# Attention and mixers in one block: the first mixer's matrix multiplies started in the last attention tiles, a second plain pair, spread seam transposes

## What is computed

```python
q_assign = argmax(einsum('bhsd,hcd->bhsc', q_n, c_n)); k_assign = argmax(... k_n ...)
scores = where(q_assign == k_assign, scale * q @ k.T, -1e9)       # B=2, H=8, S=768, D=64, 16 clusters
x = softmax(scores) @ v                                            # then [B, S, 512]
# first mixer (rank 32, hidden 2048)
u = x + (xT @ U @ V).T ;  x = u + relu(u @ w_ch1) @ w_ch2
# second mixer (token width 256, hidden 1536)
u = x + (relu(xT @ w_tok1) @ w_tok2).T ;  out = u + relu(u @ w_ch1) @ w_ch2
```

## Time and profile before

| | |
|---|---|
| median of 3 runs | 805.26 us (804.04 to 806.67) |
| profiled execution | 807.81 us, span 806.0 us |
| PE busy | 760.1 us (94%) |
| DVE, ACT, POOL busy | 555.3, 383.0, 229.7 us |
| mean granted PE clock | 0.989 of full |

### The profile page before, as it was taken

How to read it: one execution, slowest core, us unless ns; L and a number is a source line. 1 busy time by engine, 2 the same in 40 slices (tenths; PEclk the granted TensorE clock), 3 DMA queues, 4 the chain that set the end, 5 groups by cost and what they waited for, 6 DMA issues and landing times.

```text
span 806.0 us, 12514 instructions
## 1 busy us (share of the span) xinstructions
PE 760.1 (94%) x4189; PEld 680.9 (84%) x4189; DVE 555.3 (69%) x876; ACT 383.0 (48%) x709; POOL 229.7 (29%) x258
## 2 busy tenths in 40 slices
PE   6889999999999769999989999999899999889998
PEld 6778999999999659888978788988688888678987
...
DMA packets 64043, 66.65 MB, mean 83 GB/s; under 512 B 6400, under 2 KB 53824, under 8 KB 64000
## 3 DMA queue, kind: packets, MB, share of 16 engines
...
## 4 chain that ended last, share of the span: by engine, by line
PE 58%; DVE 4%; ACT 3%; issue 1%; ACTq 0%
PE bank L1193 27%; PE bank L1176 21%; PE bank L1157 3%; PE bank L1124 2%; PE bank L1109 2%; PE bank L1140 1%; ACT uT L1259 1%; DVE a_lo L1372 1%; ACT bc_hi L1252 1%; DVE x L1385 1%; DVE bc_lo L1395 0%; DVE w_lo L1424 0%; ACT a_hi L1245 0%; PE bank L1096 0%; DVE kT_hi L1429 0%
## 5 line engine op out<-in xcount | busy, mean ns | idle before, releaser
L1292 ACT ACTIVATE qT_hi<-h 128x768 fp32r<-128x768 f32 x48 | 40.6, 847 | 281.6 <-DVE h L1439 223.4
L1193 PE MATMUL bank<-w_hi,qT_hi 128*128 128x512 f32 x336 | 132.4, 394 | 1.8 <-DVE x L1380 1.7
L1193 PE MATMUL bank<-w_hi,kT_hi 128*128 128x512 f32 x336 | 133.4, 397 | 0.0
L1193 PE MATMUL bank<-w_lo,qT_hi 128*128 128x512 f32 x336 | 132.7, 395 | 0.0
L1176 PE MATMUL bank<-bc_hi,a_hi 128*128 128x384 f32 x336 | 112.4, 335 | 3.0 <-DVE kT_hi L1411 1.7
L1176 PE MATMUL bank<-bc_lo,a_hi 128*128 128x384 f32 x336 | 113.1, 337 | 0.0
L1176 PE MATMUL bank<-bc_hi,a_lo 128*128 128x384 f32 x336 | 112.3, 334 | 0.0
L629 DVE TENSOR_TENSOR pT_lo<-back,pT_hi 128x384 fp32r<-128x384 f32 x192 | 98.0, 552 | 6.7 <-ACT pT_hi L530 3.5
L530 ACT ACTIVATE pT_hi<-back 128x384 fp32r<-128x384 f32 x192 | 84.3, 497 | 35.6 <-PE back L774 33.6
L1031 POOL TENSOR_TENSOR a_raw<-a_raw 128x256 f32<-128x256 f32 x24 | 20.5, 856 | 282.5 <-DMA a_raw<-in_moe_w_ch_dram 281.3
L1439 DVE TENSOR_TENSOR h<-bank,h 128x384 f32<-128x384 f32 x120 | 64.4, 553 | 51.1 <-PE bank L1176 50.9
...
## 6 DMA issues: line engine op xcount, KB each, us to landing
...
```

Of the source, the lines that this page charges most:

```text
L1193: last = nc.tensor.matmul(acc[k][:, :], y[:, e, k * P:(k + 1) * P], w[n % 2][:, e, :], start=(start and i == 0), stop=(stop and i == 2))
L1292: nc.scalar.activation(hs_hi[:, e, :], h[:, e, :], ACT.Relu).then_inc(hs_hi_made, 1)
```

## The change

All of it in one block: `attention` and `mixers` now return one function for each engine, which `program` calls one behind the other, so that nothing joins the engines between them. Semaphores live as long as the block. `U_st` (the split U) has a place of its own. The mixers' parts for ACT, DVE and PE are cut into `head`, `middle`, `tail` and `rest`; the first ones are called inside the attention's last tiles (`mix`). The diff, cut to its core:

```diff
+        if last and t == TPP - 2:
+            steps.append(("MIX", 0, 0))
     if last:
-        steps += [("F", GPP - 2, 0)] + [("AV", GPP - 1, part) for part in range(AV_PARTS)] + [("F", GPP - 1, 0)]
+        steps += [("F", GPP - 2, 0), ("MIX", 1, 0)] + [("AV", GPP - 1, part) for part in range(AV_PARTS)]
+        steps += [("MIX", 2, 0), ("F", GPP - 1, 0)]
...
-                                pool.wait_ge(head_in[j], PAIRS * HEAD_LOADS)
-                        if G > 0:
+                                pool.wait_ge(head_in[j], (PAIRS if g is NPAIR - 3 else NPAIR - 2) * HEAD_LOADS)
+                            if g is NPAIR - 2:
+                                pool.wait_ge(uv_in, 5 * 16)
+                                split_V()
+                        else:
                             split_x(0, (g - NPAIR + 3) * GT + G - 1)
                     if last_pair:
                         if G == 0:
                             for j in range(2):
                                 pool.wait_ge(head_in[j], NPAIR * HEAD_LOADS)
-                            pool.wait_ge(uv_in, 5 * 16)
                             split_U()
-                        elif G == 1:
-                            split_V()
                         else:
-                            if G == 2:
+                            if G == 1:
                                 pool.wait_ge(x_done, (NPAIR - 1) * GPP)
-                            for i in range(GT * (G - 2), GT * (G - 1)):
+                            for i in range(2 * G - 2, 2 * G):
                                 split_x(1, i)
...
+                    if last_pair and t == TPP - 2:
+                        mix[0]()
                 if last_pair:
                     fin(GPP - 2)
+                    mix[1]()
...
+                    if last_pair and t == TPP - 1:
+                        mix[0]()
                     low(t, 0)
                     low(t, 1)
                     if first_pair and t == 0:
                         first_link(LAST)
                 if last_pair:
+                    mix[1]()
                     group(GPP - 1)
...
+    PLAIN = (2, 1, 1, 1)
...
-            return acc[t - 2] if cc == 0 and t >= 2 else ring_bank(cc, t)
+            return acc[t] if cc == 0 else ring_bank(cc, t)
...
-                if n == 1:
+                if n == 2:
...
-            pair_sums(1)
+            pool.wait_ge(tok_mm, B)
...
+                    pe.wait_ge(uT_made, t + 1)
+                elif t == 2:
+                    pe.wait_ge(exp_done, NPAIR * TPP)
+                elif t == 4:
+                    pe.wait_ge(p_lo, NPAIR * TPP * 2)
...
+                if p > 0 or g >= 2:
+                    pe.wait_ge(group_made, plain_at(n) + g - 1)
+                elif cc > 0:
+                    pe.wait_ge(uT_made, cc * NT + NT - 1 + g)
+                elif g == 0:
+                    pe.wait_ge(p_lo, NPAIR * TPP * 2)
                 else:
-                    pe.wait_ge(group_made, 4 * cc + g - 1)
+                    pe.wait_ge(fin_copied, NPAIR * GPP)
...
-                if start and k == 0:
-                    wait(pe, y_made, cc * NT)
-                    pe.wait_ge(u_made, min(cc + 2, NCH) * NT)
+                if start:
+                    wait(pe, y_made, (cc - 1) * NT + k + 1)
+                    pe.wait_ge(u_made, NT + k + 1 if cc == 0 else min(cc + 2, NCH) * NT)
...
+            def head():
+                token_first_low(0)
+
+            def middle():
+                for t in range(GT):
+                    token_second_low(0, t)
+
+            def tail():
+                for t in range(GT):
+                    transpose_u(0, t)
+                for t in range(GT, NT):
+                    token_second_low(0, t)
+
+            def rest():
+                group(0, 0, 0)
+                for t in range(GT, NT):
+                    transpose_u(0, t)
+                group(0, 0, 1)
+                token_first_low(1)
+                group(0, 0, 2)
+                for t in range(GT):
+                    token_second_low(1, t)
+                group(0, 0, 3)
+                for t in range(GT, NT):
+                    token_second_low(1, t)
+                for cc in range(NCH):
+                    if cc > 0:
+                        for g in range(len(GROUPS)):
+                            group(cc, 0, g)
+                            if cc in MIXED:
+                                for t in ((), (0,), (1, 2), (3, 4, 5))[g]:
+                                    token_first(cc, t)
+                    for p in range(1, PLAIN[cc]):
+                        for g in range(len(GROUPS)):
+                            group(cc, p, g)
+                            for unit in range(3 * g, 3 * g + 3):
+                                down(cc, p - 1, unit)
+                    for p in range(PLAIN[cc], npair[cc]):
+                        mixing = cc in MIXED and p == PLAIN[cc]
+                        units = iter(range(len(UNITS)))
+                        for q in range(BLOCKS):
+                            product(cc, p, q)
+                            if mixing and q == 1:
+                                for t in range(NT):
+                                    token_second(cc, t)
+                            if q > int(mixing):
+                                for unit in [next(units) for _ in range(4 if mixing and q == BLOCKS - 1 else 2)]:
+                                    down(cc, p - 1, unit)
+                    for unit in range(len(UNITS)):
+                        if cc + 1 < NCH:
+                            for t in {0: (0, 1), 2: (2,), 4: (3,), 6: (4,), 8: (5,)}.get(unit, ()):
+                                transpose_u(cc + 1, t)
+                        down(cc, npair[cc] - 1, unit)
+
+            return head, middle, tail, rest
...
+            def head():
+                a_high(0)
+                t1_high(0)
+
+            def tail():
+                for t in range(GT):
+                    block_high(0, t)
+
+            def rest():
+                for t in range(GT):
+                    uT_copy(0, t)
+                late = slice(DM - 2 * D, DM)
+                act.wait_ge(x_done, NPAIR * GPP)
+                nc.scalar.activation(x_hi[:, NT:2 * NT, late], x[:, :, DM + late.start:DM + late.stop],
+                                     ACT.Copy).then_inc(x_hi_made, 1)
+                group_high(0, 0)
+                for t in range(GT, NT):
+                    block_high(0, t)
+                group_high(0, 1)
+                a_high(1)
+                t1_high(1)
+                for t in range(GT, NT):
+                    uT_copy(0, t)
+                group_high(0, 2)
+                group_high(0, 3)
+                for e in range(2):
+                    w2_high(0, e)
+                group_high(0, 0, 1)
+                t_high(0, 0)
+                group_high(0, 1, 1)
+                t_high(0, 1)
+                for e in range(2):
+                    w2_high(1, e)
+                group_high(0, 2, 1)
+                t_high(0, 2)
+                a_high(2)
+                group_high(0, 3, 1)
+                t_high(0, 3)
+                for cc in range(NCH):
...
-                    t_high(cc, 0)
-                    t_high(cc, 1)
-                    group_high(cc, 0)
-                    a_high(n + 1)
-                    t_high(cc, 2)
-                    group_high(cc, 1)
                     for e in range(2):
                         w2_high(n, e)
+                    a_high(n + 1)
+                    group_high(cc, 0)
+                    t_high(cc, 0)
+                    group_high(cc, 1)
+                    t_high(cc, 1)
                     group_high(cc, 2)
+                    t_high(cc, 2)
                     group_high(cc, 3)
                     t_high(cc, 3)
...
+            def head():
+                a_low(0, 0)
+                t1_low(0)
+
+            def tail():
+                for t in range(GT):
+                    add_mix(0, t)
+
+            def rest():
+                for t in range(GT):
+                    block_low(0, t)
+                for t in range(GT, NT):
+                    add_mix(0, t)
+                late = slice(DM - 2 * D, DM)
+                dve.wait_ge(x_hi_made, 1)
+                nc.vector.tensor_tensor(x_lo[:, NT:2 * NT, late], x[:, :, DM + late.start:DM + late.stop],
+                                        x_hi[:, NT:2 * NT, late].bitcast(F32), ALU.subtract).then_inc(x_made, 1)
+                group_low(0, 0)
+                for t in range(GT, NT):
+                    block_low(0, t)
+                group_low(0, 1)
+                a_low(1, 0)
+                t1_low(1)
+                group_low(0, 2)
+                for t in range(GT):
+                    add_mix(1, t)
+                group_low(0, 3)
+                for t in range(GT, NT):
+                    add_mix(1, t)
+                w2_low(0)
+                group_low(0, 0, 1)
```

(25 more changed lines are left out.)

426 lines of the change are left out of this document (193 added, 233 removed).

## The result

The changed kernel takes 796.92 us in the median of four runs (795.7 to 797.63), the kernel before 805.24 beside it: ratio 0.9894, 95% interval 0.9872 to 0.9916. The change saves 8 to 10 us. The forecast was 788.8, with 784 to 796 as its range: the sign was right, the size was twice what came.

What follows compares the result with a forecast made beforehand. PE was taken to be bound by waits between attention and first woven pair, and at the seams. Savings of 12.6 + 1.8 + 0.4 + 1.7 = 16.5 us from 807.81, less 2.55 for the median, gave 788.8; range 784 to 796.

Steps and rivals of the forecast that it cites:

- Term 1: From the attention's end to pair 2's first product, 59.8 us before: predicted to save 12.6 us.
- the waits of 1.5 and 2.0: PE was to wait 1.5 us for DVE's token work and 2.0 for pair 2's low weights before its first product.
- the overlap does not overlap: Rival, 0.05: PE stands at the inserted token product; term 1 gives about 5 us, not 12.6; 797 to 799.
- The 1.33 of PE behind a weight split of 3.26 stays: PE's 1.33 us wait was to remain, since POOL's conversions move a pair on together with the pairs.
- The rival on POOL and DVE: Rival, 0.10: in the plain pair POOL stretches DVE's weight split to 5.6 us from 2.09; 793.
- The clock should stay at full, since no wait reaches the two beside which it fell: Behind the attention, expected waits were shorter than 2.71 and 3.91 us, so the clock was to stay full.
- The clock rival: Rival, 0.12: the clock falls again behind the attention, at waits of 1.5 and 2.0; gain 4 us less, 792.8.
- Seams: Chunks 1 and 2: 0.9 us saved at each ahead of the first down, plus 0.4 at the seam to chunk 1.
- the rule for mixed pairs: In chunks 1 and 2 a product stands between token step and first down, saving 0.9 us each.
- the whole 0.8 of the first seam: Transposes at the seam to chunk 1 took 6.51 us against 5.69 at the next; half the difference, 0.4, was forecast saved.
- the rest is given back: At the seams of chunks 1 and 2, groups start 2.8 us sooner, but DVE and POOL leave 0 of it.
- Last seam: Seam to chunk 3: DVE's new order was to end the last plain group's low part 1.7 us sooner.

Runs made afterwards that it cites:

- x9: The kernel of x6 with the mixer's head, middle and tail put behind the whole attention on PE, ACT and DVE: 786.54 us, ratio 0.9745.
- x6: The changed kernel with the edits of x1 and x2, the last seam's group low parts before x additions, and an earlier `V_raw` copy on ACT: 785.51 us.
- x7: The changed kernel with one plain pair in chunk 0 instead of two, pair 1 being woven: 800.8 us, ratio 0.9932.
- x1: The changed kernel with pair 2's low weights split on DVE ahead of the last plain group's low part: 791.2 us, ratio 0.9805.
- x4: The changed kernel with ACT's and DVE's order at the seam to chunk 3 as in the kernel before: 796.86 us, ratio 0.9868.
- x2: The changed kernel with both token-weight conversions on POOL held back until DVE has split the next pair's channel weights: 791.18 us, ratio 0.9805.
- x8: The changed kernel with the seams' transposes one down unit apart again, not two: 799.22 us, ratio 0.9898.
- x12: The kernel of x6 with the seams' transposes one down unit apart again: 788.27 us, ratio 0.9757.

## Why the prediction was wrong

**Term 1, 12.6: right in size, wrong in its cause.** 12.0 came; the waits of 1.5 and 2.0 were 1.37 and 1.96, the first plain group started at 275.54 ("near 275"), pair 2's product at 310.16 ("near 309"). But the rival "the overlap does not overlap" put 7 to 8 of the 12.6 on the overlap. By x9, on the kernel of x6, it is worth 2.1. That the measured time stands where this rival's did (797 to 799) is chance: it had term 1 at 5. The rest is the order behind and the join that is gone, which no run separates: what was late for PE before now stands behind plain groups, and x7 shows the second plain pair alone at 7.8 at this point of the program.

**"The 1.33 of PE behind a weight split of 3.26 stays": this step failed.** I moved POOL's conversions with the pairs, which is what they did, and left out what they meet. Before, the first conversion, 6.15 us of it, met DVE when it was on time, and cost PE nothing; only the second one cost 1.33. The second did move on with its pair, as I said: 0.73 in pair 3 (1.70 in x1, 2.42 in x4). The first met a late DVE and cost the 1.78. My own wait of 2.0 ahead of pair 2 was the sign that something is late there, and I stopped following it at PE's product. Behind it PE ran at the lower clock, DVE waited for PE's third product, and its next splits came 1.7 us later against POOL's conversion than before (6.9 for 5.2 us behind the pair's first product). By these distances it is the fall, more than the wait, that brought them together; no execution has the wait without the fall, so that is read and not tested. x1 and x2 show the meeting itself from both sides. The rival on POOL and DVE had the mechanism, but one pair too early, at the split near 306, where POOL was idle.

**"The clock should stay at full, since no wait reaches the two beside which it fell": this step failed too,** and cost the most: 4.9 us, where the whole stretch behind the landmark fell 5.3 short of 16.5. I made a bound out of two waits, 2.71 and 3.91, and it did not hold in the very trace I took it from: there the clock also fell behind the 1.82 at the seam to chunk 1 (0.79 from 420 to 428). In the changed kernel it fell behind 1.96, 1.78 and 3.38. That it fell because of the waits is shown by their removal: x1, x2, x4 and x6 take seven of them away, and at none of the seven places a fall is left. Restarts apart, the two steps make 4.5 of the 4.7 us lost in pairs 2 and 3 (1.78 and 0.73 of waits less the 1.33 before, 3.3 of clock) and 1.6 at the last seam. By x4 the two are not independent: without the fall behind the 1.78 its 1.6 would have been a longer wait for DVE in pair 3. The rivals on the clock (4 us) and on POOL and DVE (3.5) were each given as the only thing to go wrong, and they came together, the one helped by the other. The clock rival's own sum was short too: the falls of before lie from 275.4 to 278.7 and from 295.9 to 302.6, with only 0.6 us of the wait of 3.91 in them, so 4.7 us were lost there, not 3.5.

**Seams.** Forecast 2.2 for chunks 1 and 2, 3.0 came: 1.0 and 1.1 by the rule for mixed pairs (0.9 forecast), and the whole 0.8 of the first seam, of which I took half. But that 0.8 (6.51 for 5.69 us of transposes) was the fall of the clock in before's trace, not the spacing: x8, with close transposes and no fall, has 5.68 there and loses nothing, x12, with a fall, has the 0.8 again. That the rest is given back held to 0.02 us (x8). **Last seam:** 1.7 forecast, 1.0 came, and not by DVE's order, as my working had it: the spread transposes brought 2.3 (30.23 to 27.90 in x4), the new order lost 1.35 of it. I had counted DVE's queue to the second product's group, and not asked what stood ahead of the first one's: four additions to x and a low block, 3.4 us, while the group's high part had been ready since 698.7.

**The rest** is scatter that my sum took for constant: 0.7 ahead of the landmark, and the profiled execution of before lay 2.55 above its median, that of the changed kernel 0.7, so the medians differ by 1.9 less than the two executions.
